# Attention, token mixing and two channel MLPs on one core: down weights re-read from DRAM as already split, and a shifted order of matmuls

## The reference

```
scores = q k^T / 8 within |i-j| < 16, and q k_max^T / 8 + log(32) for 24 blocks of 32 keys
x      = softmax([scores]) @ [v, block means of v]                      # [2, 768, 512]
u      = x + (relu(x^T @ w_tok1) @ w_tok2)^T                            # 768 -> 256 -> 768
y      = u + relu(u @ w_ch1) @ w_ch2                                    # 512 -> 1536 -> 512
xn     = (y - mean) / sqrt(var + 1e-6) * g_ln
out    = y + relu(xn @ w2_ch1) @ w2_ch2                                 # 512 -> 2048 -> 512
```

## Time and profile before

| what | us |
|---|---|
| median of 3 runs | 611.49 (610.71 to 612.65) |
| the profiled execution: its time, its span | 611.88, 610.0 |
| TensorE busy | 585.5 (96% of the span) |
| VectorE, ScalarE, GpSimd busy | 307.9, 219.4, 215.1 |
| DMA | 94.38 MB, mean 155 GB/s |

### The profile page before, as it was taken

The page is one execution under the profiler, slowest core; times in us unless marked ns, Lnnn a source line. Parts: engine busy times, 40 slices in busy tenths (PEclk is TensorE's granted clock), DMA queues, the critical chain, the costliest instruction groups (busy, mean ns, idle before and its releaser), DMA issues.

```text
span 610.0 us, 8249 instructions
## 1 busy us (share of the span) xinstructions
PE 585.5 (96%) x2976; PEld 497.9 (82%) x2976; DVE 307.9 (50%) x678; ACT 219.4 (36%) x420; POOL 215.1 (35%) x208
## 2 busy tenths in 40 slices
PE   6889999999999999999998999999999999999997
PEld 2677888878888888888887888888888888888886
DVE  5486656395343445763233677333444644434334
ACT  3477564553333342322326233343325212122220
POOL 4456464214443476000324944444646200000000
PEclk9899999999999999999999999999999999999999
DMA  8878630145544383443413255455318334344602
GB/s 233 240 220 220 188 106 6 51 173 190 189 182 136 108 312 143 156 155 124 152 35 125 100 190 189 156 189 190 156 75 300 132 138 145 143 156 155 225 0 104
DMA packets 26912, 94.38 MB, mean 155 GB/s; under 512 B 7820, under 2 KB 8056, under 8 KB 23288
## 3 DMA queue, kind: packets, MB, share of 16 engines
q1 hardware_dynamic: 26320, 93.41, 44.4%
q10 hardware_dynamic: 552, 0.44, 0.3%
HBM read 64.42 MB, written 28.84 MB: 153 GB/s over the span
## 4 chain that ended last, share of the span: by engine, by line
PE 72%; DVE 14%; issue 6%; ACT 5%; DMA 2%; POOL 1%; SPq 0%; DVEq 0%; POOLq 0%; ACTq 0%
PE bank L553 68%; DVE bank L1074 4%; ACT hidden L903 4%; DVE hidden L1066 2%; DVE u L1154 2%; PE bank L656 1%; DMA k_sb<-k_w 1%; DVE in_t L991 1%; PE bank L586 1%; DVE u L1141 1%; PE bank L587 1%; PE bank L588 1%; DMA v_far<-v_mean 1%; DVE neg_scores L1009 1%; DVE down_w L991 1%
## 5 line engine op out<-in xcount | busy, mean ns | idle before, releaser
L553 PE MATMUL bank<-down_w,hidden 128*128 128x512 f32 x1008 | 272.7, 398 | 0.0
L553 PEld LDWEIGHTS bank<-down_w,hidden 128*128 128x128 f32 x1008 | 186.5, 189 | 26.9
L903 ACT ACTIVATE hidden<-bank 128x384 fp32r<-128x384 f32 x112 | 55.1, 492 | 279.3 <-DVE bank L1074 170.1
L553 PE MATMUL bank<-in_t,up_even 128*128 128x384 f32 x588 | 121.0, 341 | 5.3 <-DVE hidden L1066 3.2
L553 PE MATMUL bank<-in_t,up_odd 128*128 128x384 f32 x588 | 121.5, 342 | 1.6 <-DVE hidden L1066 1.4
L553 PEld LDWEIGHTS bank<-in_t,up_even 128*128 128x128 f32 x588 | 104.4, 188 | 19.4 <-DVE hidden L1066 8.1
L1066 DVE SCALAR_TENSOR_TENSOR hidden<-bank,hidden 128x384 fp32r<-128x384 f32 x112 | 62.5, 558 | 109.8 <-ACT hidden L903 109.8
L553 PEld LDWEIGHTS bank<-in_t,up_odd 128*128 128x128 f32 x588 | 104.3, 188 | 16.5 <-DVE hidden L1066 6.9
L1124 DVE TENSOR_TENSOR u<-bank,p 128x384 f32<-128x384 f32 x28 | 15.6, 557 | 101.3 <-PE bank L553 101.3
L1074 DVE TENSOR_TENSOR bank<-bank,u 128x384 f32<-128x384 f32 x84 | 47.0, 559 | 2.9
L553 PE MATMUL bank<-k_sb,q_sb 128*128 128x364 f32 x96 | 39.1, 492 | 5.3 <-POOL k_sb L421 2.8
(11 more groups left out here) (91 smaller groups left out, 593.0 us busy)
## 6 DMA issues: line engine op xcount, KB each, us to landing
raw_down<-w_ch SPq DMA_DIRECT2D x28, 512.0 KB, 3.3
up_kept<-up_even SPq DMA_DIRECT2D x7, 1792.0 KB, 8.1
up_kept<-up_odd SPq DMA_DIRECT2D x7, 1792.0 KB, 8.1
up_even<-up_kept SPq DMA_DIRECT2D x7, 1792.0 KB, 7.4
up_odd<-up_kept SPq DMA_DIRECT2D x7, 1792.0 KB, 7.2
raw_up<-w_ch SPq DMA_DIRECT2D x14, 512.0 KB, 4.2
k_sb<-k_w SPq DMA_DIRECT2D x16, 273.0 KB, 4.4
v_own<-v_w SPq DMA_DIRECT2D x8, 390.0 KB, 3.4
```

The source lines that it names most:

```text
L553: return nc.tensor.matmul(dst, lhs, rhs, start=start, stop=stop, skip_group_check=True)
L903: nc.scalar.activation(hidden[:, q % 2, f, 0, h * HN:(h + 1) * HN], src, ACT.Relu).then_inc(hid_high, 1)
```

## The change

Three parts. The first concerns the down weights: in the made groups SP now also stores the split tile `down_w` (1,024 KB, `keep_down`, DRAM tensor `down_kept`), and in the repeated groups `load_again_down(q)` reads it back into `down_w`; `high_down` and `low_down` are issued for made pairs only. The raw down weights of pairs 12 and 13 are loaded in group 0. The second is the tables: fewer down units behind the first ups of a pair and more behind the last ones, the turned batches and the GpSimd sums of group 2 one pair later, the square root of group 2 one pair later. The third is the order on the engines: `high_sums` ahead of the second `high_hidden` (except in the first pair of a group), `normed` moved from VectorE to ScalarE as an activation with scale and bias, and around pair 0 the last tile's transposes, the token-mixing products and their additions one step later.

```diff
-DOWNS_AFTER = {0: (2, 2, 2, 2, 1, 1, 2), 2: (2, 2, 1, 1, 1, 1, 1, 1, 2), 3: (2, 1, 1, 1, 1, 1, 1, 1, 1, 2)}
+DOWNS_AFTER = {0: (1, 1, 2, 2, 2, 2, 2), 2: (1, 1, 1, 1, 2, 2, 2, 1, 1), 3: (1, 1, 1, 1, 1, 2, 2, 1, 1, 1)}
-BATCHES_AT = ((0, 2, 2, 2, 2, 0), (0, 0, 3, 3, 2, 0), (0, 0, 2, 2, 2, 2, 0, 0), (0,) * 8)
-T_AT = (4, 4, 5)
+BATCHES_AT = ((0, 2, 2, 2, 2, 0), (0, 0, 3, 3, 2, 0), (0, 0, 0, 2, 2, 2, 2, 0), (0,) * 8)
+T_AT = (4, 4, 6)
+SCALE_AT = {1: 1, 2: 2}
...
             def load_down(q):
                 g, j = group_of(q)
-                if q >= 2:
-                    sp.wait_ge(down_low, q - 1)
+                m = nth_made(q)
+                if m >= 2:
+                    sp.wait_ge(down_low, m - 1)
                 else:
                     sp.wait_ge(pv_done, NTILE)
                 sp.dma_start(raw_down[:, q % 2], down_v[g // 2][j]).then_inc(ld_down[q % 2], 16)
+
+            def keep_down(q):
+                sp.wait_ge(down_low, nth_made(q) + 1)
+                sp.dma_start(down_kept[nth_made(q)],
+                             down_w[:, q % 2].bitcast(F32).rearrange("p f s c -> p (f s c)")
+                             ).then_inc(kept_down[q % 2], 16)
+
+            def load_again_down(q):
+                g, j = group_of(q)
+                wait_downs(sp, q - 2)
+                last = nth_made(q - 2) if j < 2 else nth_again(q)
+                sp.wait_ge(kept_down[q % 2], 16 * (last // 2 + 1))
+                sp.dma_start(down_w[:, q % 2].bitcast(F32).rearrange("p f s c -> p (f s c)"),
+                             down_kept[nth_again(q)]).then_inc(ld_again_down[q % 2], 16)
 
             def make_group(g):
...
                     keep_up(q)
+                    keep_down(q)
                     if q + 2 < FIRST[g] + PAIRS_OF[g]:
                         load_down(q + 2)
+                    elif g == 0:
+                        load_down(FIRST[2] + q + 2 - FIRST[1])
 
             def repeat_group(g):
                 for q in range(FIRST[g], FIRST[g] + PAIRS_OF[g]):
-                    load_down(q)
+                    load_again_down(q)
                     load_again(q)
 
...
-            load_down(FIRST[2])
-            load_down(FIRST[2] + 1)
...
-            first_tile(NT - 1)
             for t in range(GT):
                 mix_hidden(1, 1, t, score_bank[0])
+            first_tile(NT - 1)
...
-                    pe.wait_ge(down_low, q + 1)
+                    if is_made(q):
+                        pe.wait_ge(down_low, nth_made(q) + 1)
+                    else:
+                        pe.wait_ge(ld_again_down[q % 2], 16 * (nth_again(q) // 2 + 1))
...
-                    if q == 0 and i < NT:
-                        last_mix(i)
+                    if q == 0 and i:
+                        last_mix(i - 1)
...
             def high_down(q):
-                act.wait_ge(ld_down[q % 2], 16 * (q // 2 + 1))
+                act.wait_ge(ld_down[q % 2], 16 * (nth_made(q) // 2 + 1))
                 if q >= 2:
                     wait_downs(act, q - 2)
+                    if is_made(q - 2):
+                        act.wait_ge(kept_down[q % 2], 16 * (nth_made(q - 2) // 2 + 1))
                 nc.scalar.copy(down_w[:, q % 2, :, 0, :], raw_down[:, q % 2]).then_inc(down_high, 1)
+
+            def normed(ln, j):
+                if j == 0:
+                    act.wait_ge(newton, 6 * (ln + 1))
+                    if ln:
+                        act.wait_ge(in_turned, 8 * (ln + 1))
+                nc.scalar.activation(to_turn[:, j, :], natural[:, NT * ln + j, :], ACT.Identity,
+                                     bias=shift[:, j:j + 1], scale=rstd[:, 3, j:j + 1]).then_inc(nat_ready, 1)
 
...
-                high_down(q)
-                if g in (1, 2) and j == 1:
+                if is_made(q):
+                    high_down(q)
+                if making and not (g and j == 0):
+                    high_sums(q + 1)
+                if scaling:
...
-                if making:
+                if making and g and j == 0:
                     high_sums(q + 1)
+                if scaling:
+                    normed(g - 1, 0)
+                    normed(g - 1, 1)
...
+            high_x(2 * NPAIR - 1)
             copy_first(NT - 1)
-            high_x(2 * NPAIR - 1)
             high_input(0, 0)
             high_input(0, 1)
             for m in range(2):
                 high_h(1, m, score_bank[1 - m])
-                high_input(0, 2 + m)
+            high_input(0, 2)
+            high_input(0, 3)
...
-                low_down(q)
+                if is_made(q):
+                    low_down(q)
```

More of the change, by code:

```diff
@@ L111, in build @@
         sums_up = sb(ctx, "sums_up", [P, 4, 2 * P])
+        gap_low = sb(ctx, "gap_low", [P, 8])
         up_even = sb(ctx, "up_even", [P, 2, 7, 2 * P], F32R)
@@ L120, in build @@
         rstd = sb(ctx, "rstd", [P, 4, NT])
+        shift = sb(ctx, "shift", [P, NT])
+        gap_high = sb(ctx, "gap_high", [P, 16])
         with ExitStack() as a:
@@ L149, in build @@
             u3 = sb(b_, "u3", [P, HN])
-            room = sb(b_, "room", [P, 616])
+            room = sb(b_, "room", [P, 608])
             raw_in = sb(b_, "raw_in", [P, C, S])
@@ L178, in build @@
         kept = [sem(f"kept{i}") for i in range(2)]
+        ld_again_down = [sem(f"ld_again_down{i}") for i in range(2)]
+        kept_down = [sem(f"kept_down{i}") for i in range(2)]
         ld_down = [sem(f"ld_down{i}") for i in range(2)]
@@ L246, in build @@
         up_w = (up_even, up_odd)
+        down_kept = nc.dram_tensor("down_kept", [NMADE, P, 2 * 2 * DM], F32, kind="Internal").ap()
         up_kept = nc.dram_tensor("up_kept", [NMADE, P, 2 * 7 * 2 * P], F32, kind="Internal").ap()
@@ L908, in pair @@
                 ending = g + 1 < NGROUP and j == PAIRS_OF[g] - 1
+                scaling = SCALE_AT.get(g) == j
                 act.wait_ge(up_done, 7 * q + 1)
@@ L940, in pair @@
                 high_hidden(q, 2, product_bank(q, 5)[:, 0:HN])
+                if scaling:
+                    normed(g - 1, 2)
+                    normed(g - 1, 3)
                 if ending:
@@ L944, in pair @@
                 high_hidden(q, 3, product_bank(q, 6)[:, 0:HN])
+                if scaling:
+                    normed(g - 1, 4)
+                    normed(g - 1, 5)
                 if ending:
@@ L1096, in row_scales @@
                 dve.wait_ge(dev_done, ln + 1)
+                if ln:
+                    dve.wait_ge(nat_ready, NT * ln)
                 nc.vector.reciprocal(r[:, 0], dev[:]).then_inc(newton, 1)
-                dve.wait_ge(newton, 5 * ln + 1)
+                dve.wait_ge(newton, 6 * ln + 1)
                 nc.vector.tensor_tensor(r[:, 1], r[:, 0], r[:, 0], ALU.mult).then_inc(newton, 1)
-                dve.wait_ge(newton, 5 * ln + 2)
+                dve.wait_ge(newton, 6 * ln + 2)
                 nc.vector.tensor_tensor(r[:, 2], r[:, 1], var[:], ALU.mult).then_inc(newton, 1)
-                dve.wait_ge(newton, 5 * ln + 3)
+                dve.wait_ge(newton, 6 * ln + 3)
                 nc.vector.tensor_scalar(r[:, 1], r[:, 2], -0.5, 1.5, ALU.mult, ALU.add).then_inc(newton, 1)
-                dve.wait_ge(newton, 5 * ln + 4)
+                dve.wait_ge(newton, 6 * ln + 4)
                 nc.vector.tensor_tensor(r[:, 3], r[:, 0], r[:, 1], ALU.mult).then_inc(newton, 1)
[L1106 to L1113, removed]
+                dve.wait_ge(newton, 6 * ln + 5)
+                nc.vector.scalar_tensor_tensor(out=shift[:], in0=moments[:, :, 0], scalar=-1.0, in1=r[:, 3],
+                                               op0=ALU.mult, op1=ALU.mult).then_inc(newton, 1)
             def pair(q):
@@ L1125, in pair @@
                 if q == 0:
+                    add_mixed(1, 0, o_bank[0])
                     low_first(4)
[L1127 to L1130, removed]
+                if g == 1 and j == 1:
+                    row_stats(0, 4)
+                    row_stats(0, 5)
+                if g == 2 and j == 1:
+                    row_stats(1, 0)
+                    row_stats(1, 1)
                 low_hidden(q, 0, product_bank(q, 2)[:, 0:HN])
                 if q == 0:
+                    add_mixed(1, 1, o_bank[1])
                     low_first(5)
-                    add_mixed(1, 2, o_bank[0])
                 if opening:
@@ L1157, in pair @@
                 if q == 0:
-                    add_mixed(1, 4, o_bank[0])
+                    add_mixed(1, 3, o_bank[1])
                 if opening:
                     add_out(g - 1, 3)
-                    if normed_group:
-                        row_stats(g - 1, 1)
-                if scaling:
-                    normed(g - 1, 0)
-                    normed(g - 1, 1)
+                    if g == 1:
+                        row_stats(0, 1)
+                if g == 2 and j == 1:
+                    row_stats(1, 3)
                 add_c(q, 1, 5, u3)
@@ L1168, in pair @@
                 if q == 0:
+                    add_mixed(1, 4, o_bank[0])
```

(34 more changed lines are left out.)

14 lines of the change are left out of this document (8 added, 6 removed).

## The result

| | us |
|---|---|
| before, median of 4 runs | 611.1 (610.52 to 612.65) |
| changed, median of 4 runs | 757.74 (755.42 to 758.62) |
| ratio of changed to before | 1.239, 95% interval 1.235 to 1.242 |
| profiled execution: its time, its span | 758.62, 756.8 |

The account below looks back on a forecast made before the run. TensorE, busy 585.5 of 610.0 us, was taken to bound the kernel. The profiled 611.9 us, plus 165 for 14 waits at 11.8 each, minus 16 of closed gaps, gave 761 us, range 742 to 784.

Parts of the forecast that it names:

- The lost head start: Repeated groups: up weights queue behind the down load's wait, head start of one pair becomes none; 14 pairs, 165 us.
- The gap: TensorE ahead of up 0 in 14 repeated pairs: stands 10.1 us per pair, bounds 6.9 and 15.5.
- The clock: TensorE behind each long gap: low granted clock costs 1.7 us each time, between 0 and 3.4.
- The gains: Small gaps on TensorE's path closed by the new order: 16 us together, between 8 and 19.
- The 0.15 us ahead of up 6: Up 6 of each pair: wait for the second hidden value goes, 28 x 0.15 = 4.2 us.
- the 0.37 us ahead of the second turn: Second turned batch of a pair: 0.37 us gap goes in 11 pairs, 4.1 us.
- the 3.9 us entry of group 2: Entry of group 2: 2.3 us idle and 1.55 us of low clock go, with earlier high_sums.
- Around pair 0 ... 1.5 us: Around pair 0: waits of 1.1 and 0.8 us get work in front of them, 1.5 us gained.
- VectorE's relief: First pairs of groups: 29 us of VectorE's time gone, shortening 4.5 us of hidden-value waits; 2.5 us gained.
- SP stores 14 x 1 MB more in the made groups ... Nothing.: Made groups: SP's added stores cost nothing, a made pair moving 3.8 MB in 17 us, half of what is possible.
- the main case: Whole kernel: 14 waits less the gains, 761 us, reaching from 744 to 780; chance 77%.
- Group 3 by 94 us longer: Sign in group 3: it takes 8 x 11.8 = 94 us more than the 8 x 16.0 of before.

Follow-up runs that it names:

- second experiment: Changed kernel with both repeated-group reads still waiting for the last down of pair q-2, but the up tile issued before the down tile: 731.45 us, one run.
- first experiment: Changed kernel with one swap: in repeated groups SP issues the up tile's read ahead of the down tile's read: 608.5 us, ratio 0.996.
- the fourth: Kernel before, with split down weights kept in DRAM and read back in groups 1 and 3, up tile issued first, old tables and order: 624.0 us, ratio 1.021.
- request ahead of the store: Changed kernel, up tile read first, and the read for each repeated group's first pair moved ahead of the last made pair's down-tile store: 595.7 us, ratio 0.974.

## Why the prediction was right

**The lost head start: right, in place, number and size.** Fourteen gaps, ahead of pairs 6 to 11 and 20 to 27, none ahead of 12 to 19. It was read from the two lists of SP, and the first two experiments show that it is the wait in front of the request that costs: with the same bytes and without that wait twelve of the gaps are gone.

**The gap: 10.1 us forecast, 9.4 measured (132 / 14).** The landing was put at 9.7 us behind the first of the two issues and is 9.0 (0.4 of issue and 8.6). The transfer in front was taken at 2.4 us, and it makes the landing 1.7 us later (9.0 against 7.3) and the gap 1.9 us longer (second experiment). The estimate from the Trainium skill, "DMA: Bandwidth & Descriptors", section "Anatomy of one DMA — SWDGE (gpsimd) path", was 8.6 us, for another path than SP's; the 9.0 measured lie nearer to it than to my 9.7.

**The clock: 1.7 us forecast, 2.1 measured (30 / 14).** Behind the one gap in the trace before, TensorE ran for 0.7 us at 2.4 GHz, and then 3.5 us at the lower level. Behind each of the 14 gaps the clock is low from the first matmul. The loss in each pair goes with the time until it rises again: 6.2 us at pair 6, where 2.9 are lost, 3.1 at pair 27, where 1.5 are lost. The two errors are of opposite sign, 0.7 us too much for the gap and 0.4 too little for the clock, and nothing in the reasoning tied them together: that 14 x 11.8 = 165 forecast comes so close to the 162 measured is in part luck.

**The gains: 16 us forecast, 15 under the gaps, 14 by themselves.** The sum was right, its terms not all. The 0.15 us ahead of up 6 and the 0.37 us ahead of the second turn are gone wherever TensorE isn't waiting for weights, as forecast, and so is the 3.9 us entry of group 2. Wrong was "Around pair 0 ... 1.5 us": there the changed kernel has three gaps, 4.7 us, where the old one had 2.8 us, and the order itself is worth nothing when tried alone. Wrong too was the weight given to VectorE's relief. It wasn't needed (the order alone gives 14 us), and pair 14 got a new gap of 2.0 us, 3.6 with the clock. The step that I didn't take was to ask what the moved `high_sums` sets going on GpSimd, and beside what on VectorE that then runs: the trace before has that contention already, in five of the 28 splits: those of pairs 5, 6, 12, 18 and 19 take 1.7 to 2.8 us instead of 1.2, each started while a GpSimd operation ran. It is also why the mean in the earlier trace rows is 1,385 ns.

**What was put at nothing.** "SP stores 14 x 1 MB more in the made groups ... Nothing." In the changed kernel it costs nothing only because a longer wait hides it. The store of the last made pair waits for VectorE's split and holds the first up tile of the next group back: 11.5 us in the first experiment, 14 in the fourth. That `keep_down` is a wait in front of a prefetch too was the same question as the main term, asked at one place and not at the other.

**The range.** The upper end of the main case is 611.9 + 182 - 16 = 778 us, not 780; nothing hangs on it.

**The signs named beforehand.** Up tiles requested within 0.5 us of the down tile: 0.42 us. Landing 9.5 us later: 8.6. Clock 0.50 behind each gap: yes. TensorE's share 79%: 80%. Group 3 by 94 us longer: from the start that pair 20 should have had (525.9) to the end of the span it is 230.9 us, where before it was 140.0 (from 470.1), 91 us more: 76 of gaps, 17 of clock, less 2 of small gaps.

## What to carry to other kernels

A queue that works in order turns the wait of its first transfer into the wait of all behind it. Before a load is put into such a list, ask for each entry behind it how much earlier than its use it was requested, and what is left of that once the new wait is met: here 17 us of head start became none, at 11.6 us for each of 14 pairs, and with two lines swapped the kernel took 608.5 us instead of 757.7. And when an operation is moved to start earlier, look at what it sets going on the engine behind it: started early in every pair, `high_sums` cost some 4 us (596.8 us against 592.5 with it early once), because GpSimd then came to lie ahead of VectorE's split.

## What the runs showed of the hardware that was not expected

- VectorE and GpSimd, each with two tensor inputs in SBUF, didn't slow each other evenly; whichever started first kept its own time. Started 0.10 us behind GpSimd's 2.40 us, VectorE's 1.21 us became 3.38; started 0.29 us ahead, VectorE kept 1.22 and GpSimd's 2.40 became 3.18. In both cases the later one is longer by what the earlier one still had to go, less 0.1 to 0.2 us. What moved between the two cases is which of the two was released first.
- A read of 1,792 KB queued behind one of 1,024 KB lands 8.6 us after its issue, against 7.3 in the earlier trace rows and 7.3 (7.0 to 7.5) in the second experiment, where it goes first. So the one in front costs it 1.3 us, and with the 0.4 us by which it is issued later the tile is 1.7 us later. The bytes in front at 444 GB/s would be 2.4 us.
- The clock's price behind nearly equal gaps of 9.2 to 9.4 us was between 1.6 and 2.9 us, by how long after the restart it stayed low (3.4 to 6.2 us).
- Behind the same gap of 2.0 us at pair 14 the granted clock fell to 0.50 in three traces (changed kernel, up tile first, new order alone), 1.6 us lost each time, and stayed at 1.00 in two (up tile first but as late, request ahead of the store). A difference of 1.6 us between two of these versions can come from that alone.
